# A 47-point transform as four small products in parts of the array, with sixteen places for its input

## What is computed

```python
X = np.fft.rfft(x, axis=1)                      # 3008 = 47 * 64 points along the sequence
Yr = X.real @ w_r - X.imag @ w_i + b_r
Yi = X.real @ w_i + X.imag @ w_r + b_i
Y  = shrink(Yr, 0.01) + 1j * shrink(Yi, 0.01)   # sign(v) * max(|v| - 0.01, 0)
y  = np.fft.irfft(Y, n=3008, axis=1).reshape(6016, 256)
h  = y @ w_in;   g = max(h, 0) + alpha * min(h, 0);   z = g @ w_out
h2 = z @ w2_in;  g2 = piecewise quadratic of h2;      out = g2 @ w2_out
```

## Time and profile before

| | |
|---|---|
| median of 3 runs | 1175.83 us (1175.59 to 1176.85) |
| profiled execution | 1175.93 us |
| its span in the trace | 1173.8 us |
| TensorE busy | 1167.1 us, 99% of the span |
| VectorE, ScalarE, GpSimd busy | 76%, 73%, 59% |
| first stage | from the start to about 34 us |

### The profile page before, as it was taken

The page is one execution under the profiler, slowest core; times in us unless marked ns, Lnnn a source line. Parts: engine busy times, 40 slices in busy tenths (PEclk is TensorE's granted clock), DMA queues, the critical chain, the costliest instruction groups (busy, mean ns, idle before and its releaser), DMA issues.

```text
span 1173.8 us, 20998 instructions
## 1 busy us (share of the span) xinstructions
PE 1167.1 (99%) x6946; PEld 1138.4 (97%) x6946; DVE 887.2 (76%) x1678; ACT 852.6 (73%) x1880; POOL 687.0 (59%) x718
## 2 busy tenths in 40 slices
PE   9999999999999999999999999999999999999998
PEld 3899999999999999999999999999999999999998
DVE  4787777777777777777777787778778787878776
ACT  3445567777676777777677688888888787878776
POOL 1017647577565767666556566665757575756554
PEclk9999999999999999999999999999999999999999
DMA  9788411111121201202005500000000000000000
GB/s 354 228 258 267 153 55 44 52 42 54 54 70 40 68 28 41 95 27 68 19 5 177 197 19 2 27 1 28 1 28 1 27 1 27 1 27 1 14 15 27
DMA packets 41644, 77.61 MB, mean 66 GB/s; under 512 B 4672, under 2 KB 21184, under 8 KB 41536
## 3 DMA queue, kind: packets, MB, share of 16 engines
q1 hardware_dynamic: 38784, 67.82, 17.5%
q10 hardware_dynamic: 2752, 8.45, 2.0%
HBM read 45.97 MB, written 30.28 MB: 65 GB/s over the span
## 4 chain that ended last, share of the span: by engine, by line
PE 99%; DVE 0%; DMA 0%; issue 0%; SPq 0%; ACT 0%
PE bank L1272 45%; PE bank L1180 39%; PE bank L1146 6%; PE bank L1165 2%; PE bank L1120 2%; PE bank L1156 2%; PE bank L1131 2%; DMA x_sb<-x 0%; DVE g_sb L985 0%; DVE y_sum L881 0%; DVE bank L970 0%; DVE y_tile L1007 0%; ACT xc_hi L653 0%; DVE r L905 0%; DVE bank L975 0%
## 5 line engine op out<-in xcount | busy, mean ns | idle before, releaser
L519 POOL TENSOR_TENSOR g_lo<-g_sb,g_hi 128x376 fp32r<-128x376 f32 x510 | 505.4, 1002 | 362.5 <-ACT g_hi L784 361.6
L1272 PE MATMUL bank<-g_hi,w_out_hi 128*128 128x376 f32 x1024 | 342.8, 335 | 0.0
L1272 PE MATMUL bank<-g_hi,w_out_lo 128*128 128x376 f32 x1024 | 341.5, 333 | 0.0
L1180 PE MATMUL bank<-xc_hi,w_in_hi 128*128 128x376 f32 x896 | 302.5, 338 | 0.1
L1180 PE MATMUL bank<-xc_hi,w_in_lo 128*128 128x376 f32 x896 | 299.6, 334 | 0.0
L1180 PE MATMUL bank<-xc_lo,w_in_hi 128*128 128x376 f32 x896 | 299.0, 334 | 0.0
L784 ACT ACTIVATE g_hi<-g_sb 128x376 fp32r<-128x376 f32 x512 | 261.1, 510 | 45.6 <-DVE g_sb L985 28.7
L1272 PE MATMUL bank<-g_lo,w_out_hi 128*128 128x376 f32 x1024 | 259.6, 334 | 0.0
L1272 PEld LDWEIGHTS bank<-g_hi,w_out_hi 128*128 128x128 f32 x1024 | 192.2, 188 | 0.5
L1272 PEld LDWEIGHTS bank<-g_hi,w_out_lo 128*128 128x128 f32 x1024 | 192.7, 188 | 0.0
L1272 PEld LDWEIGHTS bank<-g_lo,w_out_hi 128*128 128x128 f32 x1024 | 184.2, 188 | 0.0
(11 more groups left out here) (84 smaller groups left out, 1528.8 us busy)
## 6 DMA issues: line engine op xcount, KB each, us to landing
gc<-group_consts SPq DMA_DIRECT2D x24, 256.0 KB, 4.5
zt<-slots_scratch SPq DMA_DIRECT2D x24, 256.0 KB, 4.0
inverse_scratch<-v_sb SPq DMA_DIRECT2D x24, 256.0 KB, 3.3
ut<-inverse_scratch SPq DMA_DIRECT2D x16, 384.0 KB, 5.1
slots_scratch<-a_sb ACTq DMA_DIRECT2D x15, 384.0 KB, 5.6
out<-y_tile SPq DMA_DIRECT2D x30, 188.0 KB, 1.9
x_sb<-x SPq DMA_DIRECT2D x17, 256.0 KB, 6.8
prep_raw<-wpack SPq DMA_DIRECT2D x16, 256.0 KB, 2.9
```

The costliest lines, as they stand in the source:

```text
L519: pool.tensor_tensor(g_lo[kind][:, :], g_sb[n % 3][:, :], g_hi[kind][:, :].bitcast(f32), ALU.subtract)\
L1180: done = pe.matmul(bank_of[:, 0:N], w_part[:, fp, w * P:(w + 1) * P], x_part[q % 2][:, xs, :], start=first and n == 0, stop=last_one and n ...
L1272: last = pe.matmul(acc_bank[k][c][:, 0:N], w[:, fp, upper * D + c * P:upper * D + (c + 1) * P], g_part[kind][:, :], start=first and n == 0 ...
```

## The change

A tile now holds 47 rows and one of zeros for each half of n2: rows 0 to 47 of the partitions for the first half, rows 64 to 111 for the second. The stationary matrix is 48 by 64 for each half. A tile's work is four products, for each half h of n2 and each half c of the columns: the operands are in partitions 64h and up, and the result goes to partitions 64c and up of a bank. So each product uses one quarter of the array of 128 by 128. The bank is chosen by h, and one semaphore increment follows the two products of a bank. Copies move 112 partitions (`A_ROWS`) in place of 96.

There are sixteen places for the input, so no load waits for a place and nothing is cleared. Tiles 0 and 1 are loaded singly and the rest in pairs; SyncE loads the first half of each, ScalarE the second: four before its copies, the other five after the copies (and stores) of tiles 1, 3, 5, 7 and 9. Stores also cover pairs of tiles, one for each c, 384 KB each, issued by ScalarE after the copy of the pair's second tile. The sixteenth tile is in the first stage with the others. The order of rows in the scratch tensor changes, and the host permutes the constants of the 64-point transform accordingly.

```diff
-FIRST_TILES = TILES - 1
-LATE_TILES = {1: FIRST_TILES}
-X_SLOTS = 8
-PARTS = ((0, P // 2, slice(0, P, 2)), (P // 2, ROWS_PAD, slice(1, P, 4)))
+QUARTER = P // 2
+SLOTS_47 = N1 + 1
+A_ROWS = QUARTER + SLOTS_47
+LOADS = ((0, 1), (1, 1)) + tuple((t, 2) for t in range(2, TILES, 2))
+EARLY_LOADS = 4
+LATE_STORES = {2 * n + 2: (TILES_PER_BATCH + n // 2 * 2, n % 2) for n in range(TILES_PER_BATCH)}
...
+        def load_x(eng, n, h):
+            first, count = LOADS[n]
+            rows = slice(QUARTER * h, QUARTER * h + SLOTS_47)
+            eng.dma_start(x_sb[rows, first:first + count, :], x[first // 2, h, :, first % 2:first % 2 + count, :])\
+               .then_inc(x_in[n], 16)
+        def store_a(eng, t, c):
+            b, q = t // TILES_PER_BATCH, 2 * (t % TILES_PER_BATCH) + c
+            eng.wait_ge(a_left, t + 2)
+            eng.wait_ge(a_right, t + 2)
+            eng.dma_start(az_slots[b, :, q:q + 3:2, :], a_sb[QUARTER * c:QUARTER * c + SLOTS_47, t:t + 2, :])\
+               .then_inc(a_stored[b], 16)
...
+            for t in range(TILES):
                 copy_a(t, a_bank[(2 * t) % 4])
-                if t < TILES_PER_BATCH:
-                    store_a(t)
-                if t >= LEAD and t + LEAD in SCALAR_LOADS:
-                    load_rows(act, t + LEAD, 1)
+                if t % 2:
+                    if t < TILES_PER_BATCH:
+                        store_a(act, t - 1, 0)
+                        store_a(act, t - 1, 1)
+                    n = EARLY_LOADS + t // 2
+                    if n < len(LOADS):
+                        load_x(act, n, 1)
...
-            def real47(t, banks):
+            def real47(t):
+                pe.wait_ge(x_in[load_of(t)], 32)
+                for h, copied in enumerate((a_left, a_right)):
                     if t >= 2:
-                        pe.wait_ge(copied, t - 1 if t < FIRST_TILES else t)
-                    pe.matmul(banks[part][0:ROWS_PAD, :], fwd_sb[:, :], x_tile(t)[:, part * HALF_COLS:(part + 1) * HALF_COLS],
-                              start=True, stop=True).then_inc(a_done, 1)
+                        pe.wait_ge(copied, t - 1)
+                    rows = slice(QUARTER * h, QUARTER * h + SLOTS_47)
+                    for c in range(2):
+                        last = pe.matmul(a_bank[(2 * t + h) % 4][QUARTER * c:QUARTER * (c + 1), :], fwd_sb[rows, :],
+                                         x_sb[rows, t, c * HALF_COLS:(c + 1) * HALF_COLS], start=True, stop=True)
+                    last.then_inc(a_done, 1)
...
-            for t in range(FIRST_TILES):
-                real47(t, [a_bank[(2 * t + part) % 4] for part in range(2)])
+            for t in range(TILES):
+                real47(t)
             for s in range(STEPS):
                 forward(s)
-                if s in LATE_TILES:
-                    real47(LATE_TILES[s], a_bank[0:2])
```

More of the change, by code:

```diff
@@ L85, in transform_constants @@
         for half in range(HALVES):
-            fwd[half:ROWS:2, 2 * slot + half] = f
+            fwd[QUARTER * half:QUARTER * half + N1, slot] = f
             inv[2 * slot + half, half::2] = f
@@ L109, in transform_constants @@
     inv_g /= SEQ
+    place = np.arange(N2).reshape(HALVES, TILES_PER_BATCH, 2, 2).transpose(1, 2, 0, 3).reshape(N2)
+    fwd_g = fwd_g.reshape(GROUPS, 2, N2, P)[:, :, place].reshape(GROUPS, P, P)
     both = np.stack([fwd_g, inv_g], axis=2).reshape(GROUPS // 2, 2, P, 2 * P)
@@ L221, in fft_mix_ffn_kernel @@
         idle_ready = sem("idle_ready")
-        zeros_by_vector = sem("zeros_by_vector")
-        zeros_by_pool = sem("zeros_by_pool")
         wm_hi_ready = sem("wm_hi_ready")
         wm_lo_ready = sem("wm_lo_ready")
-        x_in = [sem(f"x_in{i}") for i in range(TILES)]
-        x_half_in = sem("x_half_in")
+        x_in = [sem(f"x_in{i}") for i in range(len(LOADS))]
         a_done = sem("a_done")
@@ L366, in load_u @@
                   .then_inc(u_in[t % 2], 16)
-            sp.dma_start(x_tile(0)[:, 0:HALF_COLS], x[0:P, 0:HALF_COLS]).then_inc(x_half_in, 16)
+            load_x(sp, 0, 0)
             sp.dma_start(fwd_sb[:, :], fwd47).then_inc(fwd_in, 16)
-            sp.dma_start(x_tile(0)[:, HALF_COLS:], x[0:P, HALF_COLS:]).then_inc(x_in[0], 16)
-            for t in range(FULL_TILES, TILES - 2):
-                load_x(t)
+            for n in range(1, len(LOADS)):
+                load_x(sp, n, 0)
             load_matrices(0)
[L374 to L380, removed]
+            sp.wait_ge(a_stored[0], 16 * TILES_PER_BATCH)
             load_values(0)
@@ L588, in copy_a @@
                 act.wait_ge(a_done, 2 * t + 1)
[L589 to L600, removed]
+                act.activation(a_tile(t)[0:A_ROWS, 0:HALF_COLS], bank_a[0:A_ROWS, :], ACT.Copy).then_inc(a_left, 1)
+            load_x(act, 0, 1)
             act.wait_ge(half_ready, 1)
             act.activation(neg_alpha[:, 0:1], half[:, :], ACT.Copy)
[L605 to L607 removed]
+            for n in range(1, EARLY_LOADS):
+                load_x(act, n, 1)
+            for t in range(TILES):
                 copy_a(t, a_bank[(2 * t) % 4])
[L609 to L613 removed]
+                if t % 2:
[4 more added lines that the diff above has]
+                    if n < len(LOADS):
+                        load_x(act, n, 1)
+                if t == TILES_PER_BATCH + 1:
                     act.dma_start(wm_raw[:, :], wmix).then_inc(wm_in, 16)
@@ L849, in _ @@
             dve.memset(half[:, :], 0.5).then_inc(half_ready, 1)
-            for t in VECTOR_FILLS:
-                dve.memset(x_tile(t), 0.0).then_inc(zeros_by_vector, 1)
             def copy_a(t, bank_a):
                 dve.wait_ge(a_done, 2 * t + 2)
-                dve.tensor_copy(a_tile(t)[:, HALF_COLS:], bank_a[0:ROWS_PAD, :]).then_inc(a_right, 1)
-            for t in range(FIRST_TILES):
+                dve.tensor_copy(a_tile(t)[0:A_ROWS, HALF_COLS:], bank_a[0:A_ROWS, :]).then_inc(a_right, 1)
+            for t in range(TILES):
                 copy_a(t, a_bank[(2 * t + 1) % 4])
@@ L1344 @@
         layers.append(np.concatenate([ins.reshape(FP, P, 4 * P), outs.reshape(FP, P, 2 * D)], axis=2))
-    order = list(range(0, P, 2)) + list(range(1, P, 4))
-    used = sorted(order)
-    tiles = np.zeros((TILES, P, TILE_COLS), x.dtype)
-    tiles[:, used[:ROWS]] = x.reshape(BATCH, ROWS, TILES_PER_BATCH, TILE_COLS).transpose(0, 2, 1, 3)\
-                             .reshape(TILES, ROWS, TILE_COLS)
-    rows = [tiles[:FULL_TILES].reshape(-1, TILE_COLS), tiles[FULL_TILES:, order].reshape(-1, TILE_COLS)]
+    tiles = x.reshape(BATCH, N1, HALVES, TILES_PER_BATCH // 2, 2, TILE_COLS).transpose(0, 3, 2, 1, 4, 5)
+    points = np.zeros((TILES // 2, HALVES, SLOTS_47, 2, TILE_COLS), x.dtype)
+    points[:, :, 0:N1] = tiles.reshape(TILES // 2, HALVES, N1, 2, TILE_COLS)
     fwd47, inv, group_consts = transform_constants()
-    fwd = np.zeros((P, ROWS_PAD), fwd47.dtype)
-    fwd[used] = fwd47
     rows_bias = np.concatenate([np.broadcast_to(v, (N2, D)) for v in (b_r, b_i)], axis=0)
     arrays = {
-        "x": np.concatenate(rows),
+        "x": points,
         "wmix": np.concatenate([columns(w_r), columns(w_i)], axis=1),
@@ L1361 @@
         "wpack": np.stack(layers),
-        "fwd47": fwd,
+        "fwd47": fwd47,
         "inv47": inv,
```

48 lines of the change are left out of this document (9 added, 39 removed).

## The result

The changed kernel takes **1197.25 us** (median of 4 runs, 1196.97 to 1197.74), the kernel before 1176.00 us (1175.59 to 1176.85, 4 runs). The ratio is 1.018 with a 95% interval of 1.0163 to 1.0198: 21 us slower. I had forecast 1181.5 us and a range that ended at 1192. The sign was right; the size was not, and two of the steps behind it were wrong. The one that decided it is the rate at which the input arrives.

A forecast was written before the change was run, and what follows sets the result against it. TensorE, busy 99% of the span, was taken to bound the kernel: tile 15 ending at 36.9 plus 3.15 put `mix(0)` at 40.05 against 34.38 us, +5.7 on 1175.93, so 1181.5 us; range 1172.5 to 1192 (8 in 10).

The forecast's parts named there:

- Direction and place: Whole kernel: slower (chance 0.68), the time changing by as much as the start of the first `mix`, 34.38 to 40.05 us.
- TensorE's part: First stage: at most two small products overlap, so a tile takes 1.95 us (1.72 to 2.36) instead of 1.716.
- rival (a): First stage: more than two products overlap, 0.86 us a tile, DMA bounds the stage; -2.5 us, 1173.3 us; chance 0.22.
- my two signs of being wrong: First stage: the forecast is wrong if a tile takes under 1.6 us or the clock falls below 1.00.
- A1 A2 B1 B2: Instruction order in a tile: two per product, A and B being the first half's left and right columns; B1 starts with A2.
- rival (b): First stage: only quarters with different rows overlap, six instructions or 2.57 us a tile; +15.6 us, 1191.4 us; chance 0.09.
- Loads and stores: First stage: 6.3 MB of loads and batch 0's 3.1 MB of stores at 400 GB/s add 0, up to 4 us in the range.
- Just in time: 0: First stage: tile 6's load lands at 17.3 us, TensorE wants it at 17.4, so no stall is added.
- The sixteenth tile's cover: End of first stage: `mix(0)` starts 3.15 us after tile 15's end, 0.89 of it work and 2.3 us a stall.
- ScalarE's queue: First stage: the load of tiles 6 and 7, behind two stores, is issued by 11.6 us; SyncE's queue takes half the rate.
- The sum: Whole kernel: 1175.93 + 5.7 = 1181.6, less 0.1 for the median: 1181.5 us.
- (c): First stage: no overlap of products at all, 3.43 us a tile; +29.3 us, 1205.1 us; chance 0.14.

The follow-up runs named there:

- the spread kernel: The changed kernel with each half's 48 rows of x spread over partitions as in the kernel before, clears back: 1180.38 us, ratio 1.0019 to before.
- the padded pair: The changed kernel with each half padded to 64 rows, each load writing even or odd partitions (1184.67 us), or partitions 0 to 63 or 64 to 127 (1195.60 us).

## Why the prediction was wrong

**Direction and place: right.** The time moved as the start of the first `mix` moved, 20.9 us of it in the first stage. But I forecast slower for slow products, and it came from slow loads: that the sign is right is luck.

**TensorE's part: wrong, too slow.** I wrote that "at most two lie in the array at once", since B1 stands behind A2, and took 1.95 us a tile. The traces have four instructions in 0.43 us. Weight loads of the spread kernel in a stretch at full pace (start, duration):

```profile
13.96 0.24 PEld L1102 LDWEIGHTS bank<-x_sb,fwd_sb 64*64 64x64 f32 x8 [2.70 <-issue]
14.45 0.18 PEld L1102 LDWEIGHTS bank<-x_sb,fwd_sb 64*64 64x64 f32 x4 [0.25 <-issue]
14.88 0.18 PEld L1102 LDWEIGHTS bank<-x_sb,fwd_sb 64*64 64x64 f32 x4 [0.25 <-issue]
```

Groups of four loads are 0.43 us apart, the time of one instruction of 512 columns, so a tile of eight takes 0.86 us. That was the bound of rival (a), to which I gave 0.22. A tile under 1.6 us was one of my two signs of being wrong; the other, a clock below 1.00, came too. My order A1 A2 B1 B2 doesn't hold the others up; how the chip orders the eight, the trace doesn't show. In the early rows the pace is half of that (4 loads every 0.86 us at 14.66 and 15.51 in the changed kernel) though the granted clock reads 1.00 there, as for the first tile of before. Later it is half by the clock of 0.50. So the changed kernel's own tiles hardly had the full pace: two of 2.0 us, four in 6.69, six at 1.9, four in 5.81, a mean of 1.7. That this lies near my 1.95 is luck; I had half pace for the first tile alone. The Trainium skill, TensorE: Matmul & The Clock Gate, "Part 3: Packing small matmuls — row/col tiling", has 3.07 times for four row tiles; here four quarters gave the whole factor of four where the pace was full (0.86 us for eight instructions that would take 3.43 one after another at the 0.43 us of the earlier trace rows). Its sentence that weight loads overlap only where the row group differs, which was my rival (b), would give six instructions' time a tile; the 0.86 us speak against it here.

**Loads and stores: wrong, and this is the step that failed.** I took the rate as 400 GB/s, so that tile 6 came "Just in time: 0", with 272 as the lower bound from the nearest row, for which I kept 4 us in the range. Measured were 171 GB/s from 5 to 20 us: tile 6's second half was issued at 13.27 and landed at 32.98, where I had 17.3. TensorE stood still for it from 20.4 to 33.0 us, which is most of the 15.2 us between my start of the first `mix` (40.05) and the measured one (55.23). The bound was not one: the earlier trace rows's 272 GB/s are of loads to 96 neighbouring partitions, which cover both halves of the memory, while each load of the change covers part of one half; one queue alone moved 143 GB/s that way, two at once 198. My arithmetic was off as well: 1.18 MB behind 1 MB of the other queue is 2.2 MB, which at 400 GB/s lands at 18.5 us and not 17.3, a stall of 1.1 us where the sum has 0. Spreading the same kernel's rows gave 368 GB/s and took off 17 of 21 us, and the padded pair (404 against 237) shows that the place of the rows does it. With the rows where they are, shorter runs give back 4.7 us, and single tiles perhaps 3.7 more; I had weighed neither.

I had named the rule that says so and then let it go. The Trainium skill, SBUF — State Buffer, "Door 1: The DMA port swizzle", has partitions 0 to 63 reach 8 of 16 ports. Worked out for both halves together I got an estimated 1.2 us a tile, under my 1.95. But the same page's section "Can I just issue two DMAs to hit both halves?" answers no: two such transfers at once were only 6% faster than one. Read with that, eight ports at its 27.2 GB/s are an estimated 218 GB/s for 64 rows, against 201 measured with one queue alone. For 48 rows, of which four ports take 8 each, they are an estimated 163, against 143 and 154. So far the runs agree. They don't agree on two transfers: both halves at once were 38% faster than one in runs of 8 KB (198 against 143) and 73% in runs of 4 KB (266 against 154), which is still below the spread rows. The page wants one transfer over all 128 partitions; here a transfer of 64 rows on the even partitions alone reached 418 GB/s.

**The sixteenth tile's cover: right.** The products end at 46.28 + 5.81 = 52.09 and the first `mix` starts at 55.23, 3.14 us later; I had 3.15. The stall is 2.1 to 2.2 us, forecast 2.3. What covering it would bring is 1 to 2 us by the run with tile 15 in step 1, not clear of the noise.

**ScalarE's queue: right that it is late, wrong in how.** The load of tiles 6 and 7 is late behind two stores, as worked out. But SyncE's queue didn't take "half of the rate": it took all of it until 20.4 us. The run with this load issued early takes as long, since its stores are then as late.

**The sum.** At full pace, 0.86 for 1.95 us a tile would have made the kernel some 8 us faster than forecast by my own sum (1173.3 of rival (a) for 1181.5); with loads this late the pace was halved and nothing of it showed. The measured 1197.25 lies between my rivals (b) and (c), 1191.4 and 1205.1, and neither of them happened. My range allowed 12 us for slow products and 4 for slow loads.

## What to carry to other kernels

A stage in which TensorE and the DMA engines are both near full gained nothing here from faster products: quarter products with the rows left spread gave a ratio of 0.9998. Before moving an operand's rows to suit the array, look at which partitions each single load then writes, and read the DMA share together with GB/s. A full share at 171 GB/s was here a matter of layout, not of too many bytes. A bound from a neighbouring row holds only if that row shares the property in question, here both halves of the partitions.

## What was unexpected of the hardware

- Loads of 48 neighbouring rows from two queues, one for each half: 171 and 175 GB/s in runs of 8 KB, 220 to 232 in runs of 4 KB; of 64 neighbouring rows in runs of 8 KB: 237. Rows over all partitions: 368 to 404 with the same runs of 8 KB (all from 5 to 20 us).
- One queue alone fills all 16 DMA engines at very different rates: 143 GB/s to partitions 0 to 47, 201 to partitions 0 to 63, 418 to the 64 even ones, in packets of 8 KB each time.
- Four f32 products of 48 or 64 rows by 64 columns, in four quarters of the array, run in the time of one: 8 instructions in 0.86 us at full pace. After waits, the same instructions took twice as long under a granted clock that read 1.00 as well as under 0.50.
- A transfer issued on one queue while the other has several in line moved nothing until the other had moved 1.0 to 1.4 MB more: 2.5 us with spread rows, 8.0 us in the changed kernel.
- Why runs of 8 KB are slower than runs of 4 KB where two queues load neighbouring rows (198 against 266 GB/s) is open.
